# A new order of work for the first attention units and for the attention slots of the first chunk

## What is computed

```
scores = scale * q @ [k (window of 16), block maxima of k + log 32]     2 batches, 8 heads, 768 tokens, 64 wide
a = softmax(scores);  x = a @ [v, block means of v]                     -> 1536 tokens x 512
h = relu(x @ w_in);   y = (h * h) @ w_out                               512 -> 2048 -> 512
g = y @ w2_in;        s = g * softmax(g);  out = layernorm(s) * g_ln @ w2_out    512 -> 1024 -> 512
```

## Time and profile before

| | us |
|---|---|
| median of 3 runs (503.56 to 504.85) | 503.57 |
| the profiled execution | 503.61 |
| its span | 501.8 |
| PE busy in the span | 486.9 (97%) |
| DVE, ACT, POOL busy | 249.9, 210.2, 50.0 |

### The profile page before, as it was taken

The page is one execution under the profiler, slowest core; times in us unless marked ns, Lnnn a source line. Parts: engine busy times, 40 slices in busy tenths (PEclk is TensorE's granted clock), DMA queues, the critical chain, the costliest instruction groups (busy, mean ns, idle before and its releaser), DMA issues.

```text
span 501.8 us, 8265 instructions
## 1 busy us (share of the span) xinstructions
PE 486.9 (97%) x3144; PEld 439.3 (88%) x3144; DVE 249.9 (50%) x497; ACT 210.2 (42%) x549; POOL 50.0 (10%) x75
## 2 busy tenths in 40 slices
PE   8986999998999999999999999999999999999997
PEld 6765989898999999989999999999888888888885
DVE  4865556778644444454444243445854444444440
ACT  2854656655533344443433333333443333333331
POOL 2232333340200000000000000000000000000000
PEclk9997999999999999999999999999999999999999
DMA  8997023321310100041000032121222000000101
GB/s 297 327 361 243 21 72 112 94 69 33 133 35 20 41 21 22 20 150 37 21 0 1 13 116 84 43 84 45 82 68 74 29 21 22 21 22 21 38 26 42
DMA packets 26678, 37.38 MB, mean 74 GB/s; under 512 B 2480, under 2 KB 16592, under 8 KB 26640
## 3 DMA queue, kind: packets, MB, share of 16 engines
q1 hardware_dynamic: 25808, 34.60, 21.6%
q10 hardware_dynamic: 832, 2.27, 1.3%
HBM read 30.41 MB, written 6.29 MB: 73 GB/s over the span
## 4 chain that ended last, share of the span: by engine, by line
PE 90%; DVE 5%; issue 2%; ACT 2%; POOL 0%; DVEq 0%; ACTq 0%; POOLq 0%
PE bank L846 27%; PE bank L873 24%; PE bank L992 12%; PE bank L965 12%; PE bank L788 5%; PE bank L801 3%; PE bank L835 2%; PE bank L980 2%; PE bank L882 1%; ACT probs L425 1%; PE bank L812 1%; DVE k_sum L588 1%; DVE probs L627 1%; DVE solu L745 1%; DVE probs L612 1%
## 5 line engine op out<-in xcount | busy, mean ns | idle before, releaser
L846 PE MATMUL bank<-x_hi,win_hi 128*128 128x384 f32 x256 | 89.5, 350 | 0.0
L640 DVE TENSOR_TENSOR sqr<-relu 128x384 f32<-128x384 f32 x64 | 37.6, 587 | 98.9 <-ACT relu L479 98.7
L846 PE MATMUL bank<-x_lo,win_hi 128*128 128x384 f32 x256 | 86.3, 337 | 0.0
L846 PE MATMUL bank<-x_hi,win_lo 128*128 128x384 f32 x256 | 86.3, 337 | 0.0
L873 PE MATMUL bank<-h_hi,wout_lo 128*128 128x384 f32 x256 | 85.6, 334 | 0.0
L873 PE MATMUL bank<-h_hi,wout_hi 128*128 128x384 f32 x256 | 85.5, 334 | 0.0
L873 PE MATMUL bank<-h_lo,wout_hi 128*128 128x384 f32 x256 | 85.5, 334 | 0.0
L479 ACT ACTIVATE relu<-bank 128x384 f32<-128x384 f32 x64 | 31.5, 492 | 112.9 <-PE bank L846 112.9
L846 PEld LDWEIGHTS bank<-x_hi,win_hi 128*128 128x128 f32 x256 | 48.5, 190 | 4.1 <-issue 3.3
L846 PEld LDWEIGHTS bank<-x_lo,win_hi 128*128 128x128 f32 x256 | 48.7, 190 | 0.0
L846 PEld LDWEIGHTS bank<-x_hi,win_lo 128*128 128x128 f32 x256 | 48.6, 190 | 0.0
(11 more groups left out here) (79 smaller groups left out, 739.3 us busy)
## 6 DMA issues: line engine op xcount, KB each, us to landing
win_raw<-w_in_t SPq DMA_DIRECT2D x8, 512.0 KB, 12.2
wout_raw<-w_out_t SPq DMA_DIRECT2D x8, 512.0 KB, 12.9
win_raw<-w_t SPq DMA_DIRECT2D x8, 512.0 KB, 3.4
v_ext<-vwin SPq DMA_DIRECT2D x24, 144.0 KB, 2.4
out<-o_sb SPq DMA_DIRECT2D x12, 256.0 KB, 2.0
k_raw<-kT SPq DMA_DIRECT2D x7, 400.0 KB, 4.4
q_sb<-qT SPq DMA_DIRECT2D x24, 96.0 KB, 1.9
v_next<-vblk SPq DMA_DIRECT2D x4, 384.0 KB, 4.2
```

The costliest lines, as they stand in the source:

```text
L640: nc.vector.tensor_tensor(sqr[:, n % 3, :], relu[:, n % 2, :], relu[:, n % 2, :], ALU.mult)\
L846: last = nc.tensor.matmul(up_bank(n), win[a][:, f * WC + k * P:f * WC + (k + 1) * P], x[b][:, c % 2, k * CH:(k + 1) * CH], start=(k == 0 a ...
```

## The change

Four things move; no arithmetic is added or removed.

1. PE issues `scores(8)` right behind `scores(7)`, ahead of `values(3)`, and `turned(8)` and `scores(9)` among the parts of `up(0)` and `up(1)`. Before, `scores(8)` stood among those parts, and `turned(8)` and `scores(9)` behind them as the slot of step 0.
2. On ACT and DVE the steps of units 8 and 9 move with it: `exps(8)` comes ahead of `x_high(7)`, and the squares of steps 0 and 1 (`hidden(0)`, `hidden(1)`) come ahead of `exps(9)`.
3. In chunk 0 the slots stand one and a half steps apart. Positions are now half steps: an even one is ahead of `up(n + 2)`, an odd one between `up(n + 2)` and `down(n)`. Unit u = 8 to 15 meets v at half step 3u - 22, so at steps 1, 2.5, 4, 5.5, 7, 8.5, 10 and 11.5. From chunk 1 on every position is what it was.
4. On POOL `windows_k(9)` comes ahead of `w_in_low(2)`, and `windows_k(10)` ahead of `w_in_low(3)`.

```diff
-SLOTS = {0: (None, 8, 9), 2: (8, 9, 10), 4: (9, 10, 11), 5: (10, 11, 12), 7: (11, 12, 13), 9: (12, 13, 14),
-         10: (13, 14, 15), 12: (14, 15, 16), 13: (15, 16, 17)}
+SLOTS = {3 * _u - 22: (_u, _u + 1, _u + 2) for _u in range(UPC, 2 * UPC)}
 for _u in range(2 * UPC, UNITS):
-    SLOTS[2 * (_u - UPC)] = (_u, _u + 1 if _u + 1 < UNITS else None, _u + 2 if _u + 2 < UNITS else None)
+    SLOTS[4 * (_u - UPC)] = (_u, _u + 1 if _u + 1 < UNITS else None, _u + 2 if _u + 2 < UNITS else None)
...
 # GpSimd
+            windows_k(UPC + 1)
             w_in_low(2)
+            windows_k(UPC + 2)
             w_in_low(3)
-            windows_k(UPC + 1)
...
 # ScalarE
             x_high(6)
-            w_out_high(0)
+            exps(8)
             x_high(7)
             w_in_high(2)
-            exps(8)
+            w_out_high(0)
+            copy_probsT(8)
             hidden(0)
+            copy_last(8)
             w_in_high(3)
+            hidden(1)
+            exps(9)
             w_out_high(1)
-            hidden(1)
             for n in range(STEPS):
...
+                for h in (2 * n, 2 * n + 1):
+                    if h % 2 and n + 2 < STEPS:
+                        hidden(n + 2)
+                    if h in SLOTS and SLOTS[h][1] is not None:
+                        copy_probsT(SLOTS[h][1])
...
 # VectorE
             x_low(5)
+            maxima(8)
             x_low(6)
+            normalise(8)
+            x_low(7)
             w_out_low(0)
-            x_low(7)
-            maxima(8)
-            normalise(8)
             hidden(0)
+            maxima(9)
+            hidden(1)
+            normalise(9)
             w_out_low(1)
-            hidden(1)
...
 # TensorE
             scores(7)
+            scores(8)
             values(3)
...
             values(7)
+            up(0, range(2, 3))
             up(1, range(1, 2))
-            up(0, range(2, 3))
-            scores(8)
+            turned(8)
+            up(0, range(3, 4))
+            scores(9)
             up(1, range(2, 3))
-            up(0, range(3, 4))
             up(1, range(3, 4))
             for n in range(STEPS - 2):
-                if n in SLOTS:
...
+                for j in (2 * n, 2 * n + 1):
+                    if j in SLOTS:
+                        a, b, c = SLOTS[j]
                         values(a)
...
+                    if j % 2 == 0:
+                        up(n + 2)
+                    else:
+                        down(n)
```

## The result

| | before | after |
|---|---|---|
| median | 503.56 us (6 runs, 502.32 to 504.85) | 495.65 us (6 runs, 495.47 to 498.09) |
| profiled execution, its span | 503.61, 501.8 | 495.58, 493.8 |
| PE busy | 486.9 (97%) | 482.7 (98%) |
| waits of PE for `normalise` | 5.7 us in five | none |
| first `down` starts | 48.43 us | 41.05 us |

The ratio is 0.9861 (95% interval 0.9833 to 0.9889): 7.9 us faster, where 9.1 were forecast. Of the 8.05 us that the changed kernel is ahead at step 16, 7.4 are won before the first `down` and only 0.7 in the 16 steps behind it; from there on nothing changes.

The account below looks back on a forecast made before the run. PE, busy 97% of the span, bounds the kernel, so only its stops and low clock can be won. Head 6.4 + chunk 0 2.7 = 9.1 us off 503.6 gives 494.5 us, own range 493.2 to 496.8.

Parts of the forecast that it names:

- The head: From scores(7) to the first loop steps: 6.74 us of stops plus 2.45 of low clock, less 2.8 new waits: 6.4 us.
- new waits: Stops of PE that the new order adds in the head: 1.5 + 0.5 + 0.2 + 0.3 + 0.3 = 2.8 us.
- The squares ahead of exps(9): At turned(9), reached at 44.2 us: normalise(9) ends near 44.0, so no cost, 0.2 us to spare; range 0 to 2 us.
- The lock between DVE and POOL: Shared SBUF read port: the second instruction to start waits for the whole of the first; 1.0 us taken per meeting.
- The slots of chunk 0: In chunk 0, slots one and a half steps apart remove all three waits of PE for normalise: 2.7 us.
- What is late next: Chunk 0, step 8: block sums of DVE; maxima of the next slot may be 1 us late before PE notices.
- no wait of PE between 55 and 125 us: Sign expected in the changed kernel's profile; waits for normalise in chunk 0 would mean rival 3.
- Rival 3: The chunk's waits come back elsewhere, at the block sums or an odd slot: 2.7 us lost, 497.2 us; chance 0.07.
- rival 2: The clock falls in the head all the same, at the 1.5 us stop or behind: 2.45 us, 497.0 us; chance 0.08.
- The row that spoke against it: Clock of the kernel before: 26 to 31 us stayed at 1.00 with only 3.08 us of PE work in 5.

Follow-up runs that it names:

- the head alone: The changed kernel's prologue with the old slot places of chunk 0: 496.46 us, ratio 0.9839.
- `scores(8)` further back: The changed kernel with scores(8) of PE behind values(5) instead of ahead of values(3): 496.52 us, ratio 0.9849.
- first fix: The changed kernel with w_in_low(15) of POOL ahead of the slot of step 11: 494.03 us, ratio 0.9797; run again 493.06 us.
- slots-alone: The old prologue, its slot of units 8 and 9 at step 0, with the new slot places of chunk 0: 505.2 us, ratio 1.0012.
- block-sum experiment: The changed kernel with sums_k(1, 2) of DVE at step 11 ahead of normalise(17) instead of behind it: 493.34 us, ratio 0.9794.
- both fixes: The changed kernel with w_in_low(15) of POOL ahead of the slot of step 11 and scores(8) of PE behind values(5): 492.61 us, ratio 0.9779.

## Why the prediction was right, and where it was off

The forecast was 494.5 us, measured were 495.65.

- *The head (6.4 us forecast): right, and a little better.* The first `down` came 7.4 us earlier, 7.2 without the early start of that execution (from 48.43 us in the timeline; the 48.59 of the prediction is where the chain enters that group), and the head alone measured 7.5 (503.92 against 496.46). Its mechanism was right in each part: the wait of `scores(8)` 1.46 (1.5 forecast), `values(5)` 0.65 (0.5), `values(6)` 0.20 (0.3), `scores(9)` none. Two waits that I had put in at 0.2 and 0.3, at `turned(6)` and `turned(8)`, did not come. So the new waits are 2.3 us and not 2.8, which is 0.5 of the 0.8 us; the other 0.3 I cannot split.
- *The squares ahead of exps(9) at no cost: right.* `turned(9)` was reached at 43.72 (44.2 forecast) with no stop, and `normalise(9)` had ended at 43.48, so it was as close as forecast. The lock between DVE and POOL was there as expected: `w_out_low(0)` took 1.39 us and the square of `hidden(1)` 1.36. Both stayed covered.
- *The slots of chunk 0 (2.7 us forecast): this step failed.* The three waits did go. "What is late next" I sought at the block sums of DVE and at `maxima`, and did not follow the change into POOL's list, where the slot of step 11.5 now stands in the same turn of the loop as the last `w_in_low`, and ahead of it. The term was 2.7 - 2.0 = 0.7. The order of POOL that I printed covers only the head; the same look at its end would have shown the subtract behind the last copies. Of the signs that I named, "no wait of PE between 55 and 125 us" is the one that failed. Rival 3 had this loss (2.7 us, "at the block sums") and thus nearly the place, but not the engine that passes it on.
- *The clock: rival 2 comes true in some executions, as far as the number goes.* I gave it 0.08 as if it were one fact for all; two of six runs had a low clock, at 2.4 us (2.45 forecast). That they lost it in the head is not shown: the stop in front of `up(15)` can do it too (1.4 us in the profiled run of `scores(8)` further back). In the first fix, which has stops over 0.5 us only in the head, one run was at 0.993 and some 2 us longer, so the head can probably cost as much. The row that spoke against it, full clock from 26 to 31 us, was a single execution; the slots-alone profile has the same head and falls at 30 us.

So 6.4 + 2.7 = 9.1 became 7.2 + 0.7 = 7.9. The sum missed by less than the 2.0 of its one unseen wait because the head came out 0.8 better. That the two errors had opposite signs is luck.

## What to carry to other kernels

When a table moves work in several in-order queues, go through each queue to its end and ask for every wait that moved what now stands behind it: the loss here sat on the least busy engine (10%), in a subtract that had nothing to do with the copy in front of it. In front of a wait that depends on another engine's latest result, put first what is ready and what the bound engine will need. And a stop of PE can be worth more than its length: falls of the clock cost 0.5 to 2.4 us more in some of the runs and nothing in others of the same kernel, so judge it by several executions.

## What the runs showed of the hardware

- The granted clock fell behind stops that I had thought harmless: to 0.50 from 30 us on with 2.05 us of work in the 4 us before and no stop over 1.5 us, and at 111 us behind one stop of 2.0 us after a long stretch of full work. The same kernel has it in one execution and not in the next. The amount of work from 26 to 30 us does not decide it alone: the clock fell with 2.05 us (first fix) and 2.09 us (slots alone) and stayed at full with 1.89 us (block sum) and 2.03 us (changed kernel).
- The kernel before, too, is a mixture: its runs at a mean clock of 0.996 took 502.4 to 503.0 us, at 0.993 503.2 to 504.2, at 0.989 and 0.990 503.9 to 505.3. The slots-alone profile shows one way to the lowest group, a second fall at 30 us in the head that both have.
- A DVE subtract or square with both inputs in SBUF that met a POOL subtract began its work when POOL's ended: `sqr` took 1.65 us instead of 0.55 when `w_in_low(15)` of 1.62 had started 0.4 us ahead of it (block-sum experiment). The masking, which reads PSUM and one SBUF input, took 0.52 to 0.53 us in all 32 units of each kernel.
- A small operation can meet POOL too. In the kernel before, on DVE and on POOL:

```profile
28.22 1.12 DVE L622 TENSOR_SCALAR row_den<-row_sum 128x3 f32<-128x3 f32 x1
27.85 1.46 POOL L396 COPY v_ext<-v_ext_first 24x1536 f32<-24x1536 f32 x1
```

  This addition of `normalise(6)` takes 0.17 us elsewhere; here it ends with POOL's copy, 0.95 us late. The stop of 0.90 us in front of `turned(6)` in the earlier trace rows is as long as this delay. In the changed kernel `normalise(6)` starts at 29.81, after the copy has ended at 29.10, and both are gone, which fits that `values(3)` starts 1.9 us later than before and `turned(6)` only 0.8 us later, with the 0.20 us of this execution put back. With both fixes it is 1.12 us again, under `scores(8)`, and leaves 0.3 us.
